# Two Strassen-tiled MLPs behind an attention: the orders of work of five engines rewritten, part of x's sums moved to VectorE

## What is computed

```python
# attention: q, k, v of (4, 8, 576, 64); a coarse one over means of four, and a banded one (|i-j| < 4)
out_up = np.repeat(sm_attn(mean4(q), mean4(k), mean4(v)), 4, axis=2)
out_local = softmax(where(band, scale * q @ k.T, -1e9)) @ v
x = (out_up + out_local)                                # then laid out as (2304, 512)
x = (1 / (1 + exp(-(x @ w_gate)))) * (x @ w_val) @ w_out        # first MLP, d_ff 1536
h = x @ w_in2
x = h * (1 / (1 + exp(-1.702 * h))) @ w_out2                    # second MLP, d_ff 2048
```

## Time and profile before

| | |
|---|---|
| median of 3 runs | 1040.64 us (1037.27 to 1041.56) |
| the profiled execution | 1044.47 us, of which 1042.8 us are its span |
| busy in the span: TensorE, VectorE, ScalarE, GpSimd | 915.2, 585.1, 528.3, 594.9 us |
| mean granted TensorE clock | 0.949 of full |
| moved by DMA | 184.27 MB, mean 177 GB/s |
| first matmul of the second phase | at 236.76 us |

### The profile page before, as it was taken

How to read it: one execution, slowest core, us unless ns; L and a number is a source line. 1 busy time by engine, 2 the same in 40 slices (tenths; PEclk the granted TensorE clock), 3 DMA queues, 4 the chain that set the end, 5 groups by cost and what they waited for, 6 DMA issues and landing times.

```text
span 1042.8 us, 18514 instructions
## 1 busy us (share of the span) xinstructions
PE 915.2 (88%) x6638; PEld 871.8 (84%) x6638; DVE 585.1 (56%) x1128; ACT 528.3 (51%) x1191; POOL 594.9 (57%) x483
## 2 busy tenths in 40 slices
PE   9999999997969898799898788888788888798798
PEld 7787999997868898798898788878788878788787
DVE  6677454453545555375555466555466555465476
ACT  5787645543445354355444545534545534534552
POOL 5688898897167375727365653444663444631531
PEclk9999999998989999999999999898999988898899
DMA  8775566875465946284936245335236425236321
GB/s 319 246 215 199 207 221 244 331 295 180 152 233 170 353 122 222 77 303 154 361 116 211 70 133 162 91 112 161 70 133 222 125 78 162 66 120 190 108 72 61
DMA packets 74778, 184.27 MB, mean 177 GB/s; under 512 B 5568, under 2 KB 31168, under 8 KB 71872
## 3 DMA queue, kind: packets, MB, share of 16 engines
q1 hardware_dynamic: 74688, 183.10, 51.4%
HBM read 141.66 MB, written 41.42 MB: 176 GB/s over the span
## 4 chain that ended last, share of the span: by engine, by line
PE 52%; POOL 19%; issue 10%; ACT 8%; DMA 6%; DVE 4%; SPq 1%; ACTq 0%; DVEq 0%; POOLq 0%
POOL v L2040 7%; PE o_ps L776 5%; POOL v_f L2036 5%; PE o_ps L778 5%; PE o_ps L777 5%; PE d_ps L632 4%; POOL xs_lo L2067 4%; DMA raw<-in_w_out_dram 4%; PE d_ps L633 4%; PE d_ps L634 4%; PE o_ps L623 4%; PE s_ps L632 3%; PE s_ps L634 3%; PE s_ps L633 3%; DMA job_raw<-in_w_in_dram 2%
## 5 line engine op out<-in xcount | busy, mean ns | idle before, releaser
L2040 POOL TENSOR_TENSOR v<-raw,v 128x512 fp32r<-128x512 f32 x54 | 69.3, 1283 | 247.8 <-ACT v L1028 234.2
L776 PE MATMUL o_ps<-g_hi,v 128*128 128x384 f32 x504 | 177.4, 352 | 29.8 <-DVE att L1713 29.8
L632 PE MATMUL d_ps<-xs_hi,w 128*128 128x384 f32 x360 | 128.6, 357 | 68.8 <-ACT snap L1072 44.2
L778 PE MATMUL o_ps<-g_hi,v 128*128 128x384 f32 x504 | 175.5, 348 | 0.0
L777 PE MATMUL o_ps<-g_lo,v 128*128 128x384 f32 x504 | 175.4, 348 | 0.0
L1713 DVE TENSOR_TENSOR att<-o_ps,att 128x384 f32<-128x384 f32 x212 | 117.2, 556 | 73.8 <-PE o_ps L778 72.2
L632 PEld LDWEIGHTS d_ps<-xs_hi,w 128*128 128x128 f32 x360 | 71.1, 197 | 79.2 <-ACT snap L1072 49.6
L776 PEld LDWEIGHTS o_ps<-g_hi,v 128*128 128x128 f32 x504 | 100.1, 199 | 34.6 <-POOL v L2040 18.7
L634 PE MATMUL d_ps<-xs_hi,w 128*128 128x384 f32 x360 | 125.2, 348 | 0.0
L633 PE MATMUL d_ps<-xs_lo,w 128*128 128x384 f32 x360 | 125.1, 348 | 0.0
L632 PE MATMUL s_ps<-xs_hi,w 128*128 128x384 f32 x300 | 106.0, 353 | 19.6 <-ACT snap L1078 9.4
(11 more groups left out here) (173 smaller groups left out, 2182.0 us busy)
## 6 DMA issues: line engine op xcount, KB each, us to landing
w<-w_split SPq DMA_DIRECT2D x48, 768.0 KB, 5.3
w<-w_split SPq DMA_DIRECT2D x48, 512.0 KB, 5.1
w<-w_split SPq DMA_DIRECT2D x96, 256.0 KB, 3.4
w_split<-w SPq DMA_DIRECT2D x12, 1792.0 KB, 6.7
raw<-in_w_out_dram SPq DMA_DIRECT2D x36, 512.0 KB, 6.2
w_split<-job_w SPq DMA_DIRECT2D x8, 1792.0 KB, 9.7
vw<-in_v_win_dram SPq DMA_DIRECT2D x16, 390.0 KB, 4.9
raw<-in_w_gate_val_dram SPq DMA_DIRECT2D x12, 512.0 KB, 4.0
```

The source lines that it names most:

```text
L632: pe.matmul(bank, wh[:, cols], xh[:, c, :], start=(start and c == 0), stop=False, skip_group_check=True)
L776: pe.matmul(bank, vh, gh, start=(start and k == c), stop=False, skip_group_check=True)
L778: mm = pe.matmul(bank, vl, gh, start=False, stop=(k == c + 1), skip_group_check=True)
L2040: gp.tensor_tensor(v_all[:, :, 1, v_part, :], source, v_all[:, :, 0, v_part, :], ALU.subtract).then_inc(vp_ready, 1)
```

## The change

All in the order in which instructions are called; the arithmetic of the MLPs is the same and no tile changes its size. TensorE runs `p3(b-1)` ahead of `p2(b)` and, at the end of the first phase, three outputs ahead of `p4(n)`. ScalarE's list for a pair is rewritten: the copies of the weight sums (`v_s2`, `v_s4`, `v_s3`, `v_a22`) leave the end of the pair before and stand between the snaps of the pair that uses them, `v_a11` stands ahead of `v_s1`, and the jobs' copies are split and stand later. VectorE gets the sums `T1` and `T3` of x for all phases but the first, and `T2` for the second phase (12 instructions of 128x768); they leave GpSimd. GpSimd makes the sum VS3 ahead of the rests of VS2 and VS4 (`split_pair_end`). SP issues `load_pair` in layer 2 ahead of both `fetch_12` of a pair, and two of the jobs' stores and loads one block later. The semaphores of x's sums are split by sum. ScalarE's copies of the gated values (`save11`, `save21`, `save12`) stay. Line numbers of the changed kernel are higher by 2 to 83.

```diff
-V_HIS = {VA12: 1, VS1: 2, VA11: 3, VS2: 4, VS4: 5, VS3: 6, VA22: 7}
+V_HIS = {VA12: 1, VA11: 2, VS1: 3, VS2: 4, VS4: 5, VS3: 6, VA22: 7}
...
                     fetch_12(b + 2)
                     if b == FIRST[c + 1]:
                         load_pair(c + 2)
-                    if c in (G1 + 2, G1 + 8) and b == FIRST[c + 1]:
+                    if c in (G1 + 2, G1 + 8) and b == LAST[c + 1]:
                         store_job(3 if c == G1 + 2 else 6)
                         load_job(4 if c == G1 + 2 else 7)
...
             for c in range(NL1, NG - 2, 2):
-                for b in (FIRST[c + 1], FIRST[c + 2]):
-                    fetch_3(b + 1)
-                    fetch_12(b + 2)
+                fetch_3(FIRST[c + 2])
                 load_pair(c + 2)
+                fetch_12(FIRST[c + 3])
+                fetch_3(FIRST[c + 3])
+                fetch_12(FIRST[c + 3] + 1)
...
                 p1(b)
                 p4(b - 1)
+                p3(b - 1)
                 p2(b)
-                p3(b - 1)
                 p6(b)
                 p5(b)
                 p7(b)
...
-                p4(n)
-                second(k, 3)
-                p3(n)
-                second(k, 4)
-                p1(m)
-                second(k, 5)
+                if k == 5:
+                    second(k, 3)
+                    second(k, 4)
+                    second(k, 5)
+                    p4(n)
+                    p3(n)
+                    p1(m)
...
                 snap_p1(n)
+                hi22(k)
+                hi21(k)
+                if k == 5:
+                    round_t1(1)
+                sig11(k + 1)
                 if k == 5:
                     round_t3(1)
-                hi22(k)
-                hi21(k)
-                sig11(k + 1)
                 snap_u2(n)
...
+                if k == 5:
+                    v_a12(G1)
+                    v_a11(G1)
...
+                    v_s2(c)
+                    v_s4(c)
                     snap_u2(LAST[c])
-                    v_a22(c)
                     save11(c)
                     hi11(c)
+                    v_s3(c)
+                    v_a22(c)
                     snap_u3(LAST[c])
                 snap_p1(FIRST[d])
-                if last:
-                    round_b11(q + 1)
-                    round_b21(q + 1)
...
+                snap_u2(FIRST[d])
+                hi_t1(c)
                 sig11(d)
+                if c == G1:
+                    v_s1(c)
+                snap_u3(FIRST[d])
+                hi_t3(c)
                 if c in (G1 + 2, G1 + 6, G1 + 8):
                     job_a({2: 3, 6: 5, 8: 6}[c - G1])
-                    job_s({2: 3, 6: 5, 8: 6}[c - G1])
-                snap_u2(FIRST[d])
-                save12(c)
-                hi_t1(c)
-                snap_u3(FIRST[d])
-                hi_t3(c)
                 snap_p1(LAST[d])
                 hi_t2(c)
...
-                    v_a12(c)
-                    v_s1(c)
-                    v_a11(c)
-                snap_u2(LAST[d])
-                sig12(d)
                 if c == G1:
                     v_s2(c)
                     v_s4(c)
                     v_s3(c)
                     v_a22(c)
+                if c in (G1 + 2, G1 + 6, G1 + 8):
+                    job_s({2: 3, 6: 5, 8: 6}[c - G1])
+                if last:
+                    round_t2(q + 1)
+                snap_u2(LAST[d])
+                sig12(d)
                 save11(d)
                 hi11(d)
+                if c == G1:
+                    job_a(2)
...
                 save11(d)
                 hi11(d)
                 snap_u3(FIRST[d])
-                v_a22(c)
+                hi_t2(c)
                 if last:
                     round_t1(q + 1)
+                else:
+                    v_s3(c)
+                    v_a22(c)
                 snap_p1(FIRST[n])
+                hi_t4(c)
+                if last:
+                    round_t3(q + 1)
                 gelu22(d)
-                hi_t2(c)
                 gelu21(d)
                 save21(d)
                 hi21(d)
...
                 snap_u3(FIRST[n])
+                if last:
+                    v_s2(c)
+                    v_s4(c)
                 hi_t3(d)
+                if last:
+                    v_s3(c)
...
-                v_a12(n)
+                if not last:
+                    v_a12(n)
...
                     round_b22(q + 1)
-                v_s1(n)
+                    v_a12(n)
                 v_a11(n)
+                if c == START[q] + 2 and q + 1 < len(PHASES):
+                    round_t2(q + 1)
                 save11(n)
                 hi11(n)
                 gelu22(n)
                 hi22(n)
-                v_s2(n)
-                v_s4(n)
-                if n + 2 < NG:
-                    v_s3(n)
+                v_s1(n)
 
             def last_pair(c):
...
                 low_t(k, T4, z_bank)
 
+            def wait_last(q, n):
+
+                b = LAST[START[q] - 1]
+                dve.wait_ge(in_done[b % 2], count(b, n))
+
+            def x_t2():
+
+                quarter = parts(PHASES[1][1])
+                t2 = xs_sum[ring(1, T2)][:, :, :]
+                dve.wait_ge(job_stored, 16 * JOBS_BEFORE[1])
+                vec.tensor_tensor(t2, quarter[0, 1], quarter[0, 0], ALU.subtract).then_inc(t2_step, 1)
+                dve.wait_ge(t2_step, 1)
+                vec.tensor_tensor(t2, quarter[1, 1], t2, ALU.subtract).then_inc(xsum_ready[T2], 1)
+
+            def x_t1(q):
+                quarter = parts(PHASES[q][1])
+                wait_last(q, 1)
+                vec.tensor_tensor(xs_sum[ring(q, T1)][:, :, :], quarter[0, 1], quarter[0, 0], ALU.subtract).then_inc(xsum_ready[T1], 1)
+
+            def x_t3(q):
+                quarter = parts(PHASES[q][1])
+                wait_last(q, 2)
+                vec.tensor_tensor(xs_sum[ring(q, T3)][:, :, :], quarter[1, 1], quarter[0, 1], ALU.subtract).then_inc(xsum_ready[T3], 1)
+
             def add_up(k, o):
                 q, lay, p, g = GROUPS[k]
...
+                if last:
+                    x_t1(q + 1)
                 gate21(d)
-                low22(d)
-                c11(FIRST[n])
-                low21(d)
                 c12(LAST[d])
                 gate12(d)
+                low22(d)
...
 
                 d, n = c + 1, c + 2
+                q = GROUPS[c][0]
+                last = n == START[q + 1] and q + 1 < len(PHASES)
                 c12(FIRST[c])
                 low21(c)
+                if last:
+                    x_t1(q + 1)
                 c11(FIRST[d])
                 make_t1(c)
                 make_t3(c)
...
                 low_t2(c)
                 make_t4(c)
+                if last:
+                    x_t3(q + 1)
                 c12(FIRST[d])
                 low_t4(c)
                 low21(d)
+                make_t1(d)
...
                 pool.wait_ge(vp_summed, steps + 2)
                 pair_sum(VS4, raw[:, :, V12, :], v_f[:, :, 1, VS2, :], ALU.subtract)
                 pair_low(c, VS1, v_f[:, :, 1, VS1, :])
+                pool.wait_ge(y_ready, v_free(c, VS3))
+                pair_sum(VS3, raw[:, :, V11, :], raw[:, :, V21, :], ALU.subtract)
+
+            def split_pair_end(c):
+                steps = 4 * pair(c)
                 pool.wait_ge(vp_summed, steps + 3)
                 pair_low(c, VS2, v_f[:, :, 1, VS2, :])
                 pair_low(c, VS4, v_f[:, :, 1, VS4, :])
-                pool.wait_ge(y_ready, v_free(c, VS3))
-                pair_sum(VS3, raw[:, :, V11, :], raw[:, :, V21, :], ALU.subtract)
                 pair_low(c, VS3, v_f[:, :, 1, VS3, :])
                 pair_low(c, VA22, raw[:, :, V22, :])
...
             job_lows(7)
             split_pair(G1 + 10)
+            split_pair_end(G1 + 10)
             early_x(3)
             late_x(3)
             split_pair(NL1)
             for q in range(3, len(PHASES)):
                 for c in range(START[q], START[q + 1], 2):
+                    last = q + 1 < len(PHASES) and c + 2 == START[q + 1]
+                    if last:
+                        next_t1(q + 1)
+                        next_t3(q + 1)
+                    split_pair_end(c)
                     if q + 1 < len(PHASES):
                         if c == START[q]:
                             next_b11(q + 1)
...
                             next_t2(q + 1)
-                        if c + 2 == START[q + 1]:
-                            late_x(q + 1)
+                    if last:
+                        next_t4_sums(q + 1)
+                        next_t4(q + 1)
+                        next_b22(q + 1)
                     if c + 2 < NG:
```

162 lines of the change are left out of this document (93 added, 69 removed).

## The result

| | before | after |
|---|---|---|
| median | 1041.10 us (1037.27 to 1043.60, 4 runs) | 892.63 us (891.85 to 894.23, 4 runs) |
| ratio, 95% interval | | 0.858, 0.855 to 0.861 |
| the profiled execution, its span | 1044.47, 1042.8 us | 892.45, 890.7 us |
| mean granted clock of the span | 0.949 | 0.996 |

The kernel is 148 us faster. The forecast was 906 us; the measured time is 13 us under it and inside the range.

A forecast was written before the change was run, and what follows sets the result against it. TensorE was taken as the bound, losing 182 us to idle time and slowed matmuls. Start 236.7 + floor 621 + 48 (31.3 us idle at 1.53) = 906; execution 910, median 906 us; range 885 to 955.

The forecast's parts named there:

- The signs: Layer 2 pair under 31 us, `snap_p1` wait a few us, `att` under 5, clock above 0.97, v's load before second product.
- The floor: TensorE from the second phase's first matmul: 3,588 matmuls at the full pace of 0.173 us take 621 us.
- The snaps ahead of `p6`: Pair borders: 44.2 us in 17 waits go as v roundings leave; two 0.4 us waits per pair, 13.6 us, stay.
- The second product: Layer 2: 29.8 us in 14 waits go with v's load earlier; the last pair's waits, 4.2 us, stay.
- the rival: Load of v still lands late for the second product: 27.6 us more idle, 42 us of time, 948 us; chance 13%.
- The jobs and the first pair: Jobs' copies, 9.4 us in 2 waits: 2.4 stay. First pair's waits, 8.5 and 2.0: 0 stay.
- The borders: Borders of phases: some 21 us of waits at five places; with x sums on VectorE 11 us stay.
- hindered sums: VectorE and GpSimd hinder each other at x's sums at five borders: 28 us, 934 us; chance 10%.
- The factor: Each us of TensorE idle time costs 1.53 us of time, from 182 us lost over 119 idle.

The follow-up runs named there:

- The kernel with one pause in a pair: Changed kernel with the p1 snap ahead of each layer 2 pair's second group copied in 16 pieces of 24 columns instead of one of 384: 902.34 us.
- the two parts: Kernel before with only layer 2's loads of v issued ahead of six fetches and ScalarE's v roundings between the pair's own snaps: 976.06 us, ratio 0.937.

## Why the prediction was right, and where it was off

**The signs.** Those named for being right came: a pair of layer 2 lasts 29.5 us, the wait on `snap_p1` is 1.4 us and that on `att` 2.1, the clock in layer 2 is 1.00, and the load of v is issued (597.32) ahead of the second product (600.4).

**The floor.** 621 us for 3,588 matmuls held. The second phase began 3.4 us sooner (233.3 for 236.8). That is not the change: the kernel before with the load early, whose first phase is as before, begins it at 234.0, and the difference is there at the first matmul on `o_ps`, behind the attention (124.8 for 128.3). It is about the 3.8 us by which the profiled execution of before stood above its median, so the two cancel.

**The snaps ahead of `p6`.** Right that the 44.2 us go. Undoing this step alone brings the wait back to 36.4 us, from 1.4, and costs 55 us of time. The step that failed is its remainder: "I take two waits of 0.4 us in each of 17 pairs, 13.6 us". They measured 0 in the pairs of layer 2 away from the borders, and in layer 1 1.0 in all, in six waits of 0.16 us for `g_lo`. The walk had put the margin of `snap_u2` at 0.2 us, and the trace has 0.23; I did not trust it. The kernel with one pause in a pair shows how narrow that is: 0.95 us more on ScalarE at the snap is 0.9 us more in each pair.

**The second product.** The mechanism held to the tenth: the load was put 11.5 us behind `p4` and is issued 11.5 us behind it (597.32 for 585.82). Of the waits the last pair's stay, 3.4 us for 4.2. The landing was taken at 8.0 us; here the two loads take 3.9 and 4.7 us, and the second has landed 5.1 us behind the first issue, so the cover was 4.6 us and not 1.7: the load no longer runs behind six fetches. Undoing this step adds 17.0 us of waits, not the 27.6 that the rival was priced with. The Trainium skill's fit ("DMA: Bandwidth & Descriptors", "Anatomy of one DMA") gave an estimate of 4.4 us for both loads together. The page has that fit for one DMA, issued from GpSimd; these are two, issued by SyncE, and they took the measured 5.1 us, which decides.

**The jobs and the first pair.** 2.4 us were to stay at `snap_u2`; nothing did. The walk there had GpSimd's sums 1.2 us late, and TensorE waits for no snap in these pairs. Of the first pair, put at 0, 0.5 us stay.

**The borders.** 11.1 us were forecast and some 10.1 stay: 1.24 in phase 2 for 1.5, and for 2.4 each 2.5 and 2.2 at the next two, 2.15 and 2.0 in layer 2. The sums on VectorE take 0.95 alone, as taken (1.0 to 1.1), and up to 1.63 beside GpSimd. The rival *hindered sums* is right as a mechanism and wrong in its price: it was given 28 us, with ten sums hindered; five were, and taking all the sums away gives some 4 us.

**The factor.** 31.3 us idle at 1.53 were 48 us; it was 14.9 us idle and 33 us lost to the floor, 2.2 for each. The factor came from pauses of 2 us on the mean and does not carry over to short ones. The remainder that was too high (16.4 us, 25 at 1.53) and the factor that was too low (some 10 us) cancelled in part, so it is partly luck that the time came out within 13 us. The range's lower end is not worked out rightly either: no small waits and half the border's would be 877 us, and 885 is no small waits alone.

**What was not foreseen** is where the gain comes from. The prediction named each step but treated the first two as two thirds of it. In the kernel before they bring 66 us, all of it in layer 2; some 78 of the rest need the other moves of ScalarE, GpSimd and SyncE, since in layer 1 the two parts only move the wait to the `u3` snap. By the starts of matmuls 55 us of it lie in layer 1 and some 21 at the two borders in layer 2. How they divide among the three engines, the jobs, the roundings of x and the snaps' places was not tried.
